# A fused gated-attention and mixture-of-experts kernel: four small moves in the order of its front and of unit 5

## The reference

```python
# attention, per batch and head; q, k, v, o_gate: (2, 8, 768, 40), gates: (2, 8, 768)
for t in range(S):
    m_new = max(f_gate[t] + m, i_gate[t])
    f_stab, i_stab = exp(f_gate[t] + m - m_new), exp(i_gate[t] - m_new)
    m = m_new
    C = f_stab * C + i_stab * outer(v[t], k[t])      # 40 x 40 state
    n = f_stab * n + i_stab * k[t]
    y[t] = sigmoid(o_gate[t]) * (C @ q[t]) / max(abs(n . q[t]), 1.0)
# experts, on x = y as (1536, 320); w1: (4, 320, 1024), w2: (4, 1024, 320)
p = domain_probs / (domain_probs.sum(-1) + 1e-9)
out = sum_e p[:, e] * (relu(x @ w1[e]) @ w2[e])
```

## Time and profile before

| | |
|---|---|
| runs shown | median 422.2 us of 3 (421.66 to 422.8) |
| profiled execution | 421.72 us, its span 420.0 us |
| PE busy | 412.6 us (98%) |
| DVE, ACT, POOL busy | 180.2, 159.1, 153.5 us |
| mean granted clock of TensorE | 0.995 |

### The profile page before, as it was taken

One profiled execution on the slowest core, in us unless ns is written; L12 is line 12 of the kernel. 1 busy time (PEld: TensorE's weight loads), 2 busy tenths in 40 slices (PEclk: granted clock), 3 DMA queues, 4 the chain that ended last, 5 costly groups with the idle time before them and its releaser, 6 DMA issues.

```text
span 420.0 us, 7041 instructions
## 1 busy us (share of the span) xinstructions
PE 412.6 (98%) x2706; PEld 399.3 (95%) x2706; DVE 180.2 (43%) x371; ACT 159.1 (38%) x329; POOL 153.5 (37%) x189
## 2 busy tenths in 40 slices
PE   8899999899999999999999999999999999999997
PEld 8799999899999999999999999999999999999996
DVE  5685885756554557346233132323113123131142
ACT  5375468556254745324022441143211333111111
POOL 4656835493355944404010760056100444000000
PEclk9899999999999999999999999999999999999999
DMA  8889929585532845400000232023200000010010
GB/s 237 281 268 373 393 87 334 212 310 211 194 113 70 295 139 217 153 2 1 2 0 2 70 137 70 0 70 130 77 2 0 2 0 2 0 60 5 2 62 33
DMA packets 16899, 48.45 MB, mean 115 GB/s; under 512 B 1921, under 2 KB 8594, under 8 KB 15714
## 3 DMA queue, kind: packets, MB, share of 16 engines
q1 hardware_dynamic: 16002, 45.15, 30.9%
q10 hardware_dynamic: 864, 2.84, 1.9%
HBM read 45.94 MB, written 2.05 MB: 114 GB/s over the span
## 4 chain that ended last, share of the span: by engine, by line
PE 97%; DVE 2%; issue 0%; ACT 0%; DVEq 0%
PE hid_ps L1074 41%; PE acc_ps L1093 36%; PE out_ps L1030 5%; PE score_ps L1093 3%; PE out_ps L1037 2%; PE acc_ps L1074 2%; PE score_ps L974 2%; PE add_ps L1009 1%; PE hid_ps L923 1%; PE score_ps L969 1%; PE acc_ps L1030 0%; DVE prob L739 0%; DVE h_lo L808 0%; PE out_ps L1049 0%; DVE split_qk L749 0%
## 5 line engine op out<-in xcount | busy, mean ns | idle before, releaser
L808 DVE SCALAR_TENSOR_TENSOR h_lo<-hid_ps,h_hi 128x384 fp32r<-128x384 f32 (+2 forms) x120 | 68.0, 566 | 220.3 <-ACT h_hi L585 220.2
L585 ACT ACTIVATE h_hi<-hid_ps 128x384 fp32r<-128x384 f32 (+2 forms) x120 | 59.8, 498 | 233.6 <-PE hid_ps L1074 233.6
L1093 PE MATMUL acc_ps<-w_hi,h_hi 128*128 128x320 f32 x352 | 110.4, 314 | 0.1
L1093 PE MATMUL acc_ps<-w_hi,h_lo 128*128 128x320 f32 x352 | 108.8, 309 | 0.0
L1093 PE MATMUL acc_ps<-w_lo,h_hi 128*128 128x320 f32 x352 | 108.4, 308 | 0.0
L1074 PE MATMUL hid_ps<-xt_hi,w_hi 128*128 128x384 f32 (+2 forms) x360 | 104.1, 343 | 0.1
L1074 PE MATMUL hid_ps<-xt_hi,w_lo 128*128 128x384 f32 (+2 forms) x360 | 103.8, 342 | 0.0
L439 POOL TENSOR_TENSOR w_lo<-w_raw,w_hi 128x384 fp32r<-128x384 f32 x56 | 60.7, 1086 | 117.2 <-ACT w_hi L571 117.2
L1074 PEld LDWEIGHTS hid_ps<-xt_hi,w_lo 128*128 128x128 f32 x360 | 65.4, 188 | 4.3 <-POOL w_lo L439 0.2
L1093 PEld LDWEIGHTS acc_ps<-w_hi,h_hi 128*128 128x128 f32 x352 | 66.3, 188 | 1.6 <-DVE h_lo L808 0.3
L1093 PEld LDWEIGHTS acc_ps<-w_lo,h_hi 128*128 128x128 f32 x352 | 66.2, 188 | 1.3
(11 more groups left out here) (171 smaller groups left out, 369.5 us busy)
## 6 DMA issues: line engine op xcount, KB each, us to landing
w_raw<-in_w_b SPq DMA_DIRECT2D x25, 704.0 KB, 4.2
raw<-in_qk_s SPq DMA_DIRECT2D x8, 1024.0 KB
g_all<-g_dram SPq DMA_DIRECT2D x10, 512.0 KB, 6.2
kv<-in_kv_n SPq DMA_DIRECT2D x12, 352.0 KB, 5.8
w_raw<-in_w_b ACTq DMA_DIRECT2D x3, 704.0 KB, 7.4
q_pack<-in_q_p SPq DMA_DIRECT2D x10, 192.0 KB, 6.3
out_y<-y_acc SPq DMA_DIRECT2D x12, 160.0 KB, 1.8
carry<-g_dram SPq DMA_DIRECT2D x30, 60.0 KB
```

The lines of the kernel that those rows point to most:

```text
L585: nc.scalar.activation(h_hi[:, M % RING, 0:cols], hid_bank(M)[:, 0:cols], ACT.Relu).then_inc(hid_hi, 1)
L808: nc.vector.scalar_tensor_tensor(h_lo[:, M % RING, 0:cols], hid_bank(M)[:, 0:cols], 0.0, h_hi[:, M % RING, 0:cols].bitcast(fp32), ALU.max, ...
L1093: last = nc.tensor.matmul(acc_ps[t][:, 0:DM], x, w, start=(f == 0 and i == 0), stop=(f == NF - 1 and i == 2))
```

## The change

Four edits. POOL sets the columns of unit 0 between the masks of unit 0 and the first of unit 1, and those of unit 1 between the two masks of unit 1, where both came behind the last mask. PE transposes the keys' weights behind `outputs(0)` instead of ahead of it, and does two more products of ones between `additions(0)` and `transpose_x(1)`. SP asks for weight pairs 0 and 1 behind the keys and values, where ACT did so between its exponentials. The casts of unit 5 go from slots 17 and 19 to 16 and 17, its subtractions from 19 and 21 to 18 and 19.

```diff
-CAST = {4: (11, 12), 5: (17, 19), 6: (23, 24), ...
+CAST = {4: (11, 12), 5: (16, 17), 6: (23, 24), ...
-SUB = {4: (13, 14), 5: (19, 21), 6: (25, 27), ...
+SUB = {4: (13, 14), 5: (18, 19), 6: (25, 27), ...
@@ sync, behind its first loads
+            load_pair(sp, 0)
+            load_pair(sp, 1)
             reload_scores(2)
             load_q(2)
@@ gpsimd
             causal(0, 0)
             causal(0, 1)
+            count_weights(0)
             causal(1, 0)
+            count_weights(1)
             causal(1, 1)
-            count_weights(0)
-            count_weights(1)
             unit_steps()
@@ scalar
             decays(0, 1)
-            load_pair(act, 0)
             decays(1, 0)
             decays(1, 1)
             key_exp(0)
-            load_pair(act, 1)
             split_high(0, None)
             load_pair(act, 2)
@@ tensor
             first_scores(1)
+            outputs(0)
             pe.wait_ge(g0["exp"], 1)
             pe.wait_ge(g0["w_tok"], 1)
             turn(g0, "key", acc_ps[2], U0, U0, "key_ps")
-            outputs(0)
             outputs(1)
             transpose_x(0)
             additions(0)
+            keep_clock(2)
             transpose_x(1)
```

More of the change, by code:

```diff
@@ L40 @@
 DN_FIRST, DN_END = 0, 20
-CAST = {4: (11, 12), 5: (17, 19), 6: (23, 24), 7: (26, 29), 8: (33, 35), 9: (39, 41), 10: (42, 45), 11: (49, 50)}
-SUB = {4: (13, 14), 5: (19, 21), 6: (25, 27), 7: (29, 30), 8: (35, 37), 9: (41, 43), 10: (45, 46), 11: (51, 53)}
+CAST = {4: (11, 12), 5: (16, 17), 6: (23, 24), 7: (26, 29), 8: (33, 35), 9: (39, 41), 10: (42, 45), 11: (49, 50)}
+SUB = {4: (13, 14), 5: (18, 19), 6: (25, 27), 7: (29, 30), 8: (35, 37), 9: (41, 43), 10: (45, 46), 11: (51, 53)}
 OPEN_IN = {3: (2,), 13: (4,), 14: (6,), 17: (8,), 18: (10,)}
```

## The result

The changed kernel takes 419.03 us (median of 5 runs, 417.8 to 419.47), the kernel before 421.66 (median of 5, 421.25 to 422.8). The ratio is 0.993, with a 95% interval of 0.991 to 0.9951: 2.1 to 3.8 us less. The profiled execution took 419.46 us with a span of 417.6, against 420.0. It was worked out from a kernel before of 422.2 us, which took 421.66 here, so of the 3.8 us of the sum 2.6 came by the medians and 2.4 by the spans.

What follows compares the result with a forecast made beforehand. PE, busy 412.6 of 420.0 us, was taken as the bound. Gains of 2.2 us (front) and 1.56 us (unit 5), 3.8 in all, gave 417.9 from 421.7 or 418.4 from 422.2; forecast 418.2 us, range 417.0 to 420.2.

Steps and rivals of the forecast that it cites:

- the sum: Whole kernel: 2.2 us from the earlier front plus 1.56 us from unit 5's removed wait, 3.8 us in all.
- Columns between the masks: POOL's column sets fit gaps near 10.5 and 11.5 us without moving masks; first outputs start 1.23 us earlier, at 11.50.
- The clock: PE at the first outputs: with the idle gap closed the clock stays at 2.4 GHz, saving 1.51 us.
- The rival of a fall all the same: PE's clock still drops, near 13.6 us or before 11.4, costing 1.51 us: 419.7 us, chance 0.15.
- The keys' transposition: PE, behind the first outputs: new idle piece of 0.27 us, cost 0.50 us; second outputs start at 13.86, 2.21 us earlier.
- Two products of ones: PE before the second transposition of x: they fit a 0.61 us wait, cost 0, bounds 0 and 0.5 us.
- Pairs asked for by SP: First two weight pairs, behind keys and values: direct gain 0, only cover for the earlier PE; keys and values no later.
- the slower rival: Start: the weight pairs delay the keys and values, 423.7 us at 4.5 us of delay; chance 0.03 for slower.
- The store chain: POOL's sums and SP's stores come 2.5 us earlier, PE 2.2, so no wait opens before the later weights.
- the new row on `w_lo`: Sign of failure: a new PE wait on these weights between 20 and 40 us.
- the stores or pair 3 don't come earlier: Rival at block 6: PE waits there; 420.4 us if none of the 2.2 arrives, 419.3 if half; chance 0.10.
- Unit 5's casts: Before unit 5's scores: earlier slots remove PE's wait for the second subtraction, gain 1.56 us, bounds 0 and 1.56.

Runs made afterwards that it cites:

- Experiment 6: Kernel before, order untouched, with three products of ones filling PE's gap ahead of the first outputs: 420.92 us against 421.92, ratio 0.9987.
- no_ones: Changed kernel without the two added products of ones ahead of the second transposition of x: 418.72 us against 421.92 for the kernel before.
- stores_first: Changed kernel, pair 3 before the stores, two units' gates behind pair 5, ten starting products of ones, unit 2's scores and q behind the stores: 419.75 us.
- ten_ones: Changed kernel with 10 products of ones at the start instead of 12: 419.17 us against 422.1 for the kernel before.
- clock_only: Kernel before with only three products of ones added around the keys' weights' transposition, nothing moved: 420.92 us against 421.92.
- experiment 7: Two variants of the changed kernel: without the two added products of ones, 418.72 us; with 10 products at the start instead of 12, 419.17 us.
- experiment 3: Changed kernel with weight pairs 0 and 1 asked for by ACT again: 419.62 us against 422.06 for the kernel before.
- small_late: Changed kernel with ACT's loads of two chunks' gates and the domain weights (344 KB) issued later: 419.97 us against 422.06 for the kernel before.
- experiment 1: Kernel before with only unit 5's four new cast and subtraction slots: 420.09 us against 422.06, ratio 0.9953.
- five reorderings: The variants of the changed kernel in which weight pair 3 is asked for ahead of the sums' read back: medians 418.61 to 419.75 us.
- pair3_first: Changed kernel with weight pair 3 asked for by SP ahead of the stores of the sums: 419.38 us against 421.92 for the kernel before.
- gates_late10: Changed kernel, pair 3 ahead of the stores, two units' gates issued by SP behind pair 5, 10 starting products of ones: 418.61 us against 422.1.

## Why the prediction was right, and where it was not

**Columns between the masks: right.** Forecast 10.5 and 11.5, measured 10.82 and 11.86, and 0.5 us of the start is the run's own. `outputs(0)` starts when its second product on DVE is over, as the list of waits had hidden.

**The clock: right in mechanism and size.** 1.00 in all windows from 11 to 17 us, 1.98 us for the outputs where 2.03 was used. Experiment 6 shows it apart from the order of the code: 1.6 us counted from line 941 at `up(0)`, for a term of 1.51. The rival of a fall all the same isn't seen in any of the five runs of the changed kernel, but it isn't dead: four runs of its variants, one of six of `no_ones` and three of twelve of `stores_first`, have the mean clock of the kernel before (0.995 or 0.996) and are the slowest of theirs. None of them was profiled, so where the clock fell in them is open.

**The keys' transposition: right in mechanism, a little larger.** Idle time 0.36 us where 0.27 was forecast, and the whole front 2.16 us counted from line 941 for 2.2. The prediction also let the transposition begin 0.17 us before the end of the outputs, and it was 0.07 (13.90 for 11.99 + 1.98).

**The start: not foreseen.** In the profile of after the ones took 5.49 us and in that of before 5.23, so 0.5 of the 2.2 us were gone ahead of the change, as the clock rose later in that run. It is a draw of each run and not of the change: `no_ones` and `ten_ones` have 8.65 and 7.70 at line 941, and `clock_only`, with the front of before up to there, has 9.14. As experiment 7 shows, it costs the end little while block 6 binds.

**Two products of ones: 0, not contradicted** (experiment 7).

**Pairs asked for by SP: 0, not contradicted.** Medians are not told apart (experiment 3). The keys and values did not come late, so the slower rival fell.

**The store chain: the step that failed.** The prediction said "This chain gains 2.5 us and PE gains 2.2, so no wait should open", and that the sum loses what the stores lose beyond 0.3 us. `unit_sums` gained 1.74 us, 2.24 counted from line 941; the missing 0.3 is DVE's slower scan. But the stores took 3.1 us for 1.9, a time that the prediction had silently left as it was, and reading back gained 0.55. Pair 3 was then asked for 0.55 us earlier and cast 0.74 us earlier, and PE waited 0.59 us at 31.43: the new row on `w_lo` that the prediction had named as the sign of its failing. This is the half-way case of the rival "the stores or pair 3 don't come earlier" (419.3, chance 0.10 in all) much more than the forecast, and its time is the nearer: 419.03. That the median lies in the range is owed to the room left for this rival and not to the sum.

The chain has a second step that was taken too lightly: that an issue 2.5 us earlier lands 2.5 us earlier. Between the kernels before and after the landing kept step (0.55 and 0.74 us). But with the issue 1.29 us earlier again (`ten_ones`) the cast came 0.63 us earlier, and PE waited twice. In the stretch in which the DMA is full (24 to 50 us) the prediction did not add up what has to be moved. So stores at the old 1.9 us would probably have brought some of the lost gain, but no run shows it or how much: the one run with short stores (`small_late`) had other loads put ahead of pair 3. In part the room was there: the DMA share was 0.24 from 20 to 22 us, and pair 3 asked for in time to use it brought block 8 2.2 us forward, but at the price of the sums.

**Unit 5's casts: right**, 1.56 us forecast, 1.7 by the span of experiment 1, and no other wait in its place.

**The sum.** 3.8 us forecast. In the profile 2.4: 1.56 for the casts and 0.75 for the front, rounded. The median fell by 2.6, with 2.1 to 3.8 by the interval, so the timed runs alone would still allow the full sum, and it is the traces that don't.

What stays open: how much of the 1.56 us by which pair 3 was issued earlier in `small_late` the moved 344 KB took. That ACT's queue moved 0.29 MB beside it from 24 to 26 us is shown; which packets went first is not. Nor is it shown how far casts and front add up: alone the two give 2.0 us each by their ratios, together 2.95 with an interval of 2.1 to 3.8 us, which doesn't quite reach 4.0, but each of the single gains may be anything from 1.3 to 2.7 us.

## What to carry to other kernels

A gap of the engine that sets the time can cost more than its length, as here, where 1.1 us of idle time was followed by 3.5 us at half the clock. Fill or close such a gap first; three small products in it gave 1.6 of the 2.2 us at this place, though at most 1.1 of them are seen at the end. When the front of a kernel is to come earlier by x, sum up the bytes that must land until the first waits behind it, look at the DMA share of that stretch, and give a price to a store that is read back. Here the stretch was full and the stores slower than before, and 0.75 of 1.66 us were left at the first weights that weren't there; in all five reorderings tried another reader waited in their place. Look also at the clock of every timed run and not of the profiled one alone: four runs of two variants lost it, and no trace shows them.

## What was not expected of the hardware

- The windows' granted clock is 1.00 in the first microseconds of every trace, yet the matmuls of ones there last as those at the 1.2 GHz level do. In the kernel after, in the groups of PE for 2 to 3 us and for 17 to 18 us (count, busy, mean of one):

```profile
...
L923 PE MATMUL hid_ps<-ones 128*128 128x128 f32 x6 | 1.5, 421 | 0.0
```
```profile
...
L923 PE MATMUL hid_ps<-ones 128*128 128x128 f32 x4 | 0.6, 284 | 0.0
```

  The same matmul takes 421 ns and then 284. The outputs in the kernel before took 426 ns each at a granted 0.50 and 286 in the kernel after. So at the start of these traces durations tell the clock and the column does not. The Trainium skill, "TensorE: Matmul & The Clock Gate" (What's actually happening), says that the place of a transition differs between runs; the 24 matmuls of ones took from 4.75 us (`pair3_first`) to 5.49 (after), which agrees.
- Idle time of PE did not act by its length alone. Two pieces of 0.45 and 0.65 us, behind narrow matmuls, were followed by 0.50; 1.56 us in one piece in the middle of dense work was not the earlier trace rows; nor was 0.61 us at 17.53 in the profiled execution of `no_ones`. One of its five others had a fall somewhere (experiment 7).
- The same three small stores took from 1.7 to 4.1 us from the last issue until SP could go on: 1.7 and 1.9 when issued at 19.0 and 20.1 us (`clock_only`, before), 3.1 at 18.4 in the kernel after, 4.1 at 17.4 in `gates_late10`, and 2.06 at 17.85 in `small_late`. This chain through DRAM had no fixed price in these runs.
